# Opening an attention stage: the second pair of heads stacked by transfers, the first head's scores in four banks

## The reference

```python
B, H, S, D = (4, 8, 576, 64)
scores = scale * q @ k.T                      # per head, causal mask
a = softmax(scores)                           # rows reduced by their own maximum
local = a @ v
q_p = where(q > 0, q, exp(q) - 1) + 1
mem_out = (q_p @ M_prev) / (q_p @ z_prev + 1e-6)
g = sigmoid(beta)
x = (g * mem_out + (1 - g) * local)           # 2304 tokens x 512
x = (s * relu(x @ w_in)**2 + b) @ w_out       # 512 -> 2048 -> 512
h = x @ w_in2                                 # 512 -> 1024
x = layernorm(h * softmax(h)) * g_ln @ w_out2 # 1024 -> 512
```

## Time and profile before

| | us |
|---|---|
| median of three runs | 821.64 (821.0 to 822.66) |
| profiled execution | 821.17 |
| span of the profiled execution | 819.4 |
| PE busy | 810.7 (99%) |
| DVE busy | 510.4 (62%) |
| ACT busy | 339.6 (41%) |
| POOL busy | 339.1 (41%) |

### The profile page before, as it was taken

The page is one execution under the profiler, slowest core; times in us unless marked ns, Lnnn a source line. Parts: engine busy times, 40 slices in busy tenths (PEclk is TensorE's granted clock), DMA queues, the critical chain, the costliest instruction groups (busy, mean ns, idle before and its releaser), DMA issues.

```text
span 819.4 us, 14574 instructions
## 1 busy us (share of the span) xinstructions
PE 810.7 (99%) x5630; PEld 704.2 (86%) x5630; DVE 510.4 (62%) x1052; ACT 339.6 (41%) x608; POOL 339.1 (41%) x453
## 2 busy tenths in 40 slices
PE   8999999999999999999999999999999999999998
PEld 7788888888888888888888899999998888888886
DVE  7877777776588653333433353346688977777762
ACT  6766776675422232222322232233436434333431
POOL 6667676676899930000000000005268844443300
PEclk9999999999999999999999999999999999999999
DMA  8587777866134320000000000000111000000001
GB/s 152 128 178 154 173 167 155 178 142 144 53 103 116 95 73 1 1 1 0 1 1 0 1 1 1 1 1 1 52 51 52 26 27 26 26 14 27 26 14 51
DMA packets 86371, 49.45 MB, mean 60 GB/s; under 512 B 65056, under 2 KB 73248, under 8 KB 86304
## 3 DMA queue, kind: packets, MB, share of 16 engines
q1 hardware_dynamic: 83760, 47.94, 24.3%
q10 hardware_dynamic: 2544, 0.59, 0.4%
HBM read 27.28 MB, written 4.72 MB: 39 GB/s over the span
## 4 chain that ended last, share of the span: by engine, by line
PE 96%; DVE 1%; issue 0%; ACT 0%; POOL 0%; POOLq 0%
PE ps_h L1297 8%; PE ps_y L1313 8%; PE ps_h L1298 8%; PE ps_h L1299 8%; PE ps_y L1314 8%; PE ps_y L1312 8%; PE ps_v L678 5%; PE ps_s L591 4%; PE ps_r L1766 4%; PE ps_r L1764 4%; PE ps_r L1765 4%; PE ps_hid L1701 4%; PE ps_hid L1699 4%; PE ps_hid L1700 3%; PE ps_x L657 3%; PE ps_x L658 3%
## 5 line engine op out<-in xcount | busy, mean ns | idle before, releaser
L1414 DVE TENSOR_TENSOR xT<-xT 128x512 f32<-128x512 f32 (+1 forms) x80 | 61.2, 765 | 127.7 <-ACT xT L1372 127.7
L1598 POOL TENSOR_TENSOR win<-stage,win 128x512 fp32r<-128x512 f32 x2 | 2.6, 1296 | 282.4 <-ACT win L1833 282.4
L1314 PE MATMUL ps_y<-g_hi,wout 128*128 128x512 f32 (+1 forms) x320 | 117.5, 367 | 0.0
L1313 PE MATMUL ps_y<-g_lo,wout 128*128 128x512 f32 (+1 forms) x320 | 117.5, 367 | 0.0
L1312 PE MATMUL ps_y<-g_hi,wout 128*128 128x512 f32 (+1 forms) x320 | 117.4, 367 | 0.0
L1378 ACT ACTIVATE g_hi<-xT 128x512 fp32r<-128x512 f32 (+1 forms) x80 | 47.3, 591 | 135.0 <-DVE xT L1416 135.0
L1297 PE MATMUL ps_h<-x_hi,win 128*128 128x512 f32 (+1 forms) x280 | 103.0, 368 | 0.0
L1299 PE MATMUL ps_h<-x_hi,win 128*128 128x512 f32 (+1 forms) x280 | 102.8, 367 | 0.0
L1298 PE MATMUL ps_h<-x_lo,win 128*128 128x512 f32 (+1 forms) x280 | 102.8, 367 | 0.0
L1372 ACT ACTIVATE xT<-ps_h 128x512 f32<-128x512 f32 (+1 forms) x80 | 44.3, 554 | 139.0 <-PE ps_h L1299 137.2
L1419 DVE TENSOR_TENSOR g_lo<-xT,g_hi 128x512 fp32r<-128x512 f32 (+1 forms) x80 | 65.1, 813 | 52.6 <-ACT g_hi L1378 52.6
(11 more groups left out here) (220 smaller groups left out, 1814.6 us busy)
## 6 DMA issues: line engine op xcount, KB each, us to landing
stacked<-cut SPq DMA_DIRECT2D x56, 288.0 KB, 4.8
out<-res SPq DMA_DIRECT2D x18, 256.0 KB, 2.0
v_raw<-in_v SPq DMA_DIRECT2D x32, 128.0 KB, 2.7
stage<-in_moe_w_in SPq DMA_DIRECT2D x16, 256.0 KB, 2.8
stage<-in_moe_w_out SPq DMA_DIRECT2D x16, 256.0 KB, 2.7
k_raw<-in_k SPq DMA_DIRECT2D x28, 128.0 KB, 2.6
q_raw<-in_q SPq DMA_DIRECT2D x28, 128.0 KB, 3.6
stage<-in_moe_w_in SPq DMA_DIRECT2D x4, 512.0 KB, 3.5
```

The costliest lines, as they stand in the source:

```text
L1313: pe.matmul(out, wout[:, f, HI, w], g_lo[:, r, 0:n], start=False, stop=False)
L1314: ins = pe.matmul(out, wout[:, f, LO, w], g_hi[:, r, 0:n], start=False, stop=(f == FT - 1))
L1414: dve.tensor_tensor(r, r, r, ALU.mult).then_inc(square_done, 1)
```

## The change

Pair 1 is no longer placed directly (`DIRECT = 1`). Its keys and queries are loaded into the ordinary raw tiles, rounded by ScalarE and GpSimd, cut by VectorE and GpSimd, and brought to `stacked` by `stack(1)`, which SyncE issues behind the values of pair 0. The doubling on GpSimd and the swapped transposes of pair 1 are gone.

All rows of head 0 are computed in one go: tiles 4 and 1 in `ps_s` as before, tile 3 in the first bank of `ps_x`, tiles 0 and 2 in the second, without waits on maxima between them. Head 1's first rows follow as soon as their place in `ps_s` has been reduced. The transpose of head 0's maxima is taken out of `first_rows(1)` and has its own signal; head 1's low queries move from VectorE to GpSimd. GpSimd rounds and cuts pair 1's queries ahead of `spread_maxima(0)`, and a clearing of 1.53 us (the ones of `K1`) is moved behind it. ScalarE gets `round_keys(1)` and two `repeat_queries` for pair 1 in place of eight placing copies; VectorE's `work_out_gates` moves behind the first rows of head 1. Left out below: the same functions with their pair argument taken away, and sizes of counters.

```diff
--- before.py
+++ after.py
@@ -164,9 +164,8 @@
     Q1, K1 = sb("Q1", [P, SLOTS, 2, W], F32R), sb("K1", [P, LATE, 2, W], F32R)
     pT = [sb(f"pT{s}", [P, NP]) for s in range(3)]
     THREE = NT * 3 * D
-    first_k, first_q = ([words_.rearrange("p (t three d) -> p t three d", three=3, d=D) for words_ in places]
-                        for places in ((pT[0][:, 0:THREE], all_t_mem[:, 0:THREE]),
-                                       (pT[1][:, 0:THREE], all_t_mem[:, THREE:2 * THREE])))
+    first_k, first_q = (words_[:, 0:THREE].rearrange("p (t three d) -> p t three d", three=3, d=D)
+                        for words_ in (pT[0], pT[1]))
     rm, rl = sb("rm", [P, NT, 2]), sb("rl", [P, 2, NT])
...
@@ -180,6 +179,7 @@
         return ps_v[:, :, :].rearrange("p two n -> p (two n)") if p < 2 else ps_t
 
     S_AT = [512, 512 + REST, 512 + P, 0, 0]
+    X_AT = {3: (0, 0), 0: (1, 0), 2: (1, P)}
     NEG_AT = 512 + REST + 2 * P
 
...
@@ -218,12 +218,10 @@
     def is_head(h):
         return 0 <= h < HEADS
 
-    DIRECT = 2
-    BY_ACT = [(0, "k_own0"), (0, "k_moved0"), (0, "q_hi0"), (0, "q_cut0"), (0, "q_hi1"), (0, "q_own1"),
-              (1, "k_moved0"), (1, "k_moved1"), (1, "k_own0"), (1, "q_hi0"), (1, "q_cut0"), (1, "q_hi1"),
-              (1, "k_own1"), (1, "q_own1")]
-    BY_DVE = [(0, "k_own1"), (0, "k_moved1"), (0, "q_lo0"), (0, "q_lo1"), (1, "q_lo0")]
-    K_SWAPPED, Q_SWAPPED = (1, 3), (2, 4)
+    DIRECT = 1
+    BY_ACT = ["k_own0", "k_moved0", "q_hi0", "q_cut0", "q_hi1", "q_own1"]
+    BY_DVE = ["k_own1", "k_moved1", "q_lo0"]
+    K_SWAPPED, Q_SWAPPED = 1, 2
     Q_DMAS, STACK_DMAS = 3, 2
     MINE = [slice(0, D), slice(D, P)]
...
+    def score_rows(h, t):
+
+        if h == 0 and t in X_AT:
+            bank, at = X_AT[t]
+            return ps_x[:, bank, at:at + keys[t]]
+        return ps_s[:, S_AT[t]:S_AT[t] + keys[t]]
 
...
@@ -313,6 +315,7 @@
         load_queries(2)
         load_memory()
         load_values(0)
+        stack(1)
         load_keys(3)
         load_queries(3)
         load_values(1)
...
@@ -358,25 +361,22 @@
             for s in range(1, SLOTS):
                 pool.memset(words(Q1[MINE[0], s, 1, :]), 0.0).then_inc(cleared, 1)
             pool.memset(words(K1[:, 1:LATE, :, S:W]), 0.0).then_inc(cleared, 1)
+            pool.wait_ge(cleared, POOL_CLEARS - 1)
+
+        def fill_others():
...
+            pool.wait_ge(cleared, POOL_CLEARS - 1)
+
+        def fill_others():
             pool.memset(words(K1[MINE[0], 1:LATE, 1, 0:S]), 1.0).then_inc(cleared, 1)
             pool.wait_ge(cleared, POOL_CLEARS)
 
-        def double(raw, landed):
-
-            pool.wait_ge(landed, 16 * Q_DMAS)
-            pool.wait_ge(cleared_dve, PSUM_CLEARS)
-            pool.tensor_scalar(raw[:, :, 2, :], raw[:, :, 0, :], 1.0, 1.0, ALU.mult, ALU.mult).then_inc(doubled_pool, 1)
-
-        def repeat_first(p):
-            act_placed(pool, p, "q_hi0")
-            pool.tensor_scalar(Q1[MINE[0], p, 0, 0:S], words(stacked[MINE[0], slot(2 * p), 0, 0:S]), 1.0, 1.0,
+        def repeat_first():
+            act_placed(pool, "q_hi0")
+            pool.tensor_scalar(Q1[MINE[0], 0, 0, 0:S], words(stacked[MINE[0], slot(0), 0, 0:S]), 1.0, 1.0,
                                ALU.mult, ALU.mult).then_inc(repeated, 1)
 
         def low_queries():
 
-            act_placed(pool, 1, "q_own1")
-            pool.wait_ge(qT_copied, 2)
-            pool.tensor_tensor(stacked[MINE[1], slot(3), 0, 0:S], qT[1][MINE[1], :], Q1[MINE[1], 1, 1, 0:S],
+            act_placed(pool, "q_own1")
+            pool.wait_ge(qT_copied, 1)
+            pool.tensor_tensor(stacked[MINE[1], slot(1), 0, 0:S], qT[0][MINE[1], :], Q1[MINE[1], 0, 1, 0:S],
                                ALU.subtract).then_inc(low_by_pool, 1)
 
         def round_queries(p):
@@ -449,17 +449,16 @@
                 if even and is_pair(pr + 1):
                     features(pr + 1)
 
-        double(first_k[1], k_in[1])
-        double(first_q[1], q_in[1])
-        pool.wait_ge(doubled_pool, 2)
-        repeat_first(0)
+        repeat_first()
         pool.wait_ge(repeated, 1)
         clear_others()
-        repeat_first(1)
-        pool.wait_ge(repeated, DIRECT)
-        spread_maxima(0)
         low_queries()
         pool.wait_ge(low_by_pool, 1)
+        round_queries(1)
+        cut_queries(1)
+        pool.wait_ge(q_lo_done, 1)
+        spread_maxima(0)
+        fill_others()
 
         mask_weights(0, 0)
         pool.wait_ge(tri_done, 2)
@@ -523,37 +522,35 @@
...
+        def turn_maxima(h):
+            need(pe, maxed, 4 * (h + 1))
+            return pe.transpose(ps_s[:, NEG_AT:NEG_AT + P], least[h % 2][:, :], ident[:, :])
 
         def first_rows(h):
             if h == 0:
                 pe.wait_ge(cleared, FOR_ROWS)
-            if h < 2 * DIRECT:
-                p = h // 2
-                if h == 0:
-                    act_placed(pe, 0, "q_hi1")
-                    dve_placed(pe, 0, "q_lo0")
-                elif h == 1:
-                    act_placed(pe, 0, "q_hi1")
-                    dve_placed(pe, 0, "q_lo1")
-                elif h == 2:
-                    act_placed(pe, 1, "q_cut0")
-                    dve_placed(pe, 1, "q_lo0")
-                else:
-                    act_placed(pe, 1, "q_own1")
-                    pe.wait_ge(low_by_pool, 1)
+                act_placed(pe, "q_hi1")
+                dve_placed(pe, "q_lo0")
+            elif h == 1:
+                act_placed(pe, "q_own1")
+                pe.wait_ge(low_by_pool, 1)
+                pe.wait_ge(maxed, 2)
             elif h < HEADS:
                 p = h // 2
                 pe.wait_ge(stack_landed[p % SLOTS][h % 2], 16 * STACK_DMAS * stacks_sent(p))
-            need(pe, maxed, 4 * min(h, HEADS))
-            if is_head(h - 1):
-                ins = pe.transpose(ps_s[:, NEG_AT:NEG_AT + P], least[(h - 1) % 2][:, :], ident[:, :])
+            if is_head(h - 1) and h != 1:
+                ins = turn_maxima(h - 1)
             if h < HEADS:
                 rows_of_scores(h, 4)
                 ins = rows_of_scores(h, 1)
-            ins.then_inc(scored, 1)
+            if h != 1:
+                ins.then_inc(scored, 1)
 
         def second_rows(h):
-            pe.wait_ge(maxed, 4 * h + 1)
+            need(pe, maxed, 4 * h + 1 if h > 0 else 0)
             rows_of_scores(h, 3).then_inc(scored, 1)
 
         def third_rows(h):
-            pe.wait_ge(maxed, 4 * h + 2)
+            need(pe, maxed, 4 * h + 2 if h > 0 else 0)
             need(pe, neg_done, h)
             rows_of_scores(h, 0)
             rows_of_scores(h, 2).then_inc(scored, 1)
@@ -634,9 +628,7 @@
             a, p, par = slot(h), h // 2, h % 2
             kept = KEPT[par]
             if h == 0 and c == 0:
-                pe.wait_ge(k_lo_done, 1)
-                act_placed(pe, 1, "q_hi1")
-                dve_placed(pe, 1, "q_lo0")
+                pe.wait_ge(maxed, 4)
                 pe.wait_ge(cleared, FOR_FIRST)
                 pe.wait_ge(cleared_dve, DVE_CLEARS + 1)
             if h == 2 and c == 0:
...
@@ -730,25 +722,23 @@
 
         warm_up()
         turn_keys(0)
-        turn_swapped_keys(0)
+        turn_swapped_keys()
         turn_queries(0)
-        turn_swapped_queries(0)
-        act_placed(pe, 0, "k_moved0")
-        dve_placed(pe, 0, "k_moved1")
+        turn_swapped_queries()
+        act_placed(pe, "k_moved0")
+        dve_placed(pe, "k_moved1")
         keep_warm(ps_x[:, 0, 0:P])
         first_rows(0)
-        turn_swapped_keys(1)
-        pe.wait_ge(qT_copied, 1)
-        keep_warm(ps_t[:, 0:P])
         second_rows(0)
+        third_rows(0)
+        turn_queries(1)
         turn_keys(1)
-        turn_queries(1)
-        third_rows(0)
-        turn_swapped_queries(1)
-
         first_rows(1)
-        act_placed(pe, 1, "q_hi1")
-        keep_warm(ps_x[MINE[0], 0, 0:P], 4)
+        pe.wait_ge(qT_copied, 2)
+        keep_warm(ps_t[:, 0:P], 3)
+        turn_maxima(0).then_inc(scored, 1)
+        keep_warm(ps_t[:, 0:P], 4)
+
         cross(0, 0)
         second_rows(1)
         cross(0, 1)
...
-        for p, what in BY_ACT:
-            put(p, what)
-            if what == "q_own1":
-                copy_queries(p)
-                if p == 0:
-                    open_gates()
+        for what in BY_ACT:
+            put(what)
+        copy_queries(0)
+        open_gates()
+        copy_queries(1)
+        round_keys(1)
+        feature_relu(0)
         exp_weights(0, 0)
-        feature_relu(0)
+        repeat_queries(1, 0)
         exp_weights(0, 1)
         copy_queries(2)
         exp_weights(0, 2)
         feature_exp(0)
         exp_weights(0, 3)
+        repeat_queries(1, 1)
         round_keys(2)
 
         exp_weights(1, 0)
@@ -973,9 +963,8 @@
...
@@ -1128,24 +1113,24 @@
                     scale_local(pr - 1)
 
         dve.wait_ge(cleared_dve, DVE_CLEARS + 1)
-        double(first_k[0], k_in[0])
-        double(first_q[0], q_in[0])
+        double(first_k, k_in[0])
```

(75 more changed lines are left out.)

80 lines of the change are left out of this document (35 added, 45 removed).

## The result

The changed kernel takes 824.11 us (median of 11 executions, 822.58 to 827.92), the kernel before 821.43 us; the ratio is 1.0034 with a 95% interval of 1.0025 to 1.0042. It is 2.7 us slower. The profiled execution took 824.23 us, its span 822.3 against 819.4.

What follows compares the result with a forecast made beforehand. TensorE's queue plus the opening's holes was taken as the bound. The 1.7 us gained vanish in the wait for pair 1's stack, which adds 0.9: profiled 821.17 becomes 822.1, on the median 822.5 us; 8-in-10 range 821.2 to 824.9.

Steps and rivals of the forecast that it cites:

- the likeliest case: Whole kernel: pair 1's stack delays TensorE by 0.9 us, clock stays up, median 822.5 us; chance 0.50.
- the first rival: TensorE's clock falls in the 2.75 us hole, costing 1.4 us more: 823.9 us, range 823.0 to 825.0; chance 0.30.
- What bounds the kernel: TensorE's queue of work plus few holes in the opening; opening changes pay only if the unbroken queue starts at another moment.
- T: Turn of head 1's maxima with head 2's first rows on TensorE: 20.75 us before, forecast 21.65, bounds 21.3 and 22.4.
- The opening up to the first cross product: Head 0's rows, maxima and spreading: its cross product starts at 16.25 us, 1.7 us earlier.
- The new wait: TensorE waits for pair 1's first two transfers, issued by SyncE at 16.24 us; turn of head 1's maxima 0.9 us later.
- the landing: Pair 1's first two transfers, issue to landing: 5.1 us plus 0.2 for loads under way; upper bound 5.97 + 0.2.
- After T: Behind the turn of head 1's maxima, holes keep their distance; stack 2 issued at 28.25 us, in time; cost nothing.
- The two copies added to ScalarE: Query copies, about 0.65 us each, in ScalarE's idle time around the hole: cost nothing, without that cover up to 0.5 us.

Runs made afterwards that it cites:

- the run without a stack: Changed kernel without pair 1's stack, places of heads 2 and 3 cleared early by GpSimd and used as they are; 820.10 us, ratio 0.9982 to the kernel before.
- the early stack: Changed kernel with ScalarE rounding and VectorE subtracting pair 1's queries, its stack issued ahead of pair 0's values; 824.89 us, ratio 1.0043.
- the eight fillers: Changed kernel with eight filling matmuls in TensorE's wait for pair 1's stack; 823.03 us, ratio 1.0020.
- the half stack: Changed kernel with half of pair 1's stack copied by ScalarE on its own partitions, one transfer per head left; 821.41 us, ratio 1.0007.
- the turn of the maxima apart: Kernel before, with only the transpose of head 0's maxima given its own signal and head 1's first rows behind VectorE's copy; 821.28 us, ratio 0.9996.
- twelve: Changed kernel with twelve filling matmuls in TensorE's wait for pair 1's stack; 823.64 us, ratio 1.0026.
- three or two in the half stacks: Half of pair 1's transfers with three fillers, 821.34 us; or with two, queries ready earlier, stack ahead of values, head 3's copies later, 820.13 us.
- the early stack with five: Changed kernel with pair 1's queries readied by ScalarE and VectorE, stack ahead of values, and five filling matmuls; 822.35 us, ratio 1.0016.
- the stack ahead of the values: Changed kernel with one line moved: pair 1's stack issued ahead of the loads of pair 0's values; 825.46 us, ratio 1.0048.

## Why the prediction was right or wrong

The range held the time and the direction was right, but the likeliest case was not the one that came: it said 0.9 us, measured are 2.7. What came is the first rival, and its 823.9 us against the measured 824.11 is in part luck: the landing was longer than in its sum, the price of the clock lower, and 0.3 us came from elsewhere.

*What bounds the kernel.* Right. The later T appeared at the end one for one (2.56 us at head 3's turn, 2.87 at the last turn, 2.9 of span), and so did the earlier one in the run without a stack.

*The opening up to the first cross product.* Right in mechanism and nearly in size: 16.25 forecast, 16.36 measured; counted from head 0's rows, 5.82 and 6.11 us. The 0.3 us lie between the start of the spreading and the cross product, 1.06 us instead of 0.79: the 0.79 was read at head 1, while at head 0 itself the old kernel had 1.21 us, from the row below to 17.95.

```profile
16.74 0.74 POOL L404 TENSOR_SCALAR_AFFINE_SELECT Q<-negT 5x640 fp32r<-5x640 f32 x1 [0.97 <-DVE negT L1018]
```

That GpSimd's new operations of pair 1, and not the turned maxima, hold back the spreading is in its timeline (rounding, subtraction, then the spreading at once); the maxima had been copied since 14.81:

```profile
13.06 0.67 POOL L386 TENSOR_SCALAR cut<-qT 128x576 fp32r<-128x576 f32 x1
13.82 1.41 POOL L392 TENSOR_TENSOR cut<-qT,cut 128x576 fp32r<-128x576 f32 x1
15.30 0.74 POOL L404 TENSOR_SCALAR_AFFINE_SELECT Q<-negT 5x640 fp32r<-5x640 f32 x1
```

In the early stack, where GpSimd doesn't have these two operations, the cross product came 5.81 us behind head 0's rows instead of 6.11. The 1.7 us of gain were 1.5 when measured alone (1.41 by the distance of T from head 0's rows).

*The new wait.* Right in mechanism: SyncE's queue sets the issue (15.75; the stretch of loads ahead of it ended 0.5 us sooner than in the kernel before), TensorE waits on the second transfer. The term that was mis-sized is the landing: 5.1 + 0.2 us were taken and 5.97 + 0.2 was the upper bound, 6.6 came. The bound was made from the stacks of a single trace. What the traces have for this stack is 5.07 us where nothing stood just ahead, 5.0, 5.4 and 6.6 with the values ahead, 6.3 with the memory's transfers, whose last issue ended 0.8 us ahead. What makes the difference stays open: later stacks that were issued 0.1 us behind a load of keys took 5.06 us in the changed kernel (at 42.84) and 6.3 us with the eight fillers (at 41.13), and the one of 6.5 us in the changed kernel had 1.1 us free ahead of it. So the 0.2 us should have been a spread of 0 to 1.5. By the estimate from the Trainium skill ("DMA: Bandwidth & Descriptors", section "Anatomy of one DMA"), 3.4 us for both transfers, the miss would have been larger.

*After T.* The distances between T and what follows were kept within 0.1 us, as forecast, where the clock stayed up; the half stack, with its two more copies, lost the 0.4 us told above. The two copies added to ScalarE cost nothing. The prediction put that down to the hole as cover, without which they could cost up to 0.5 us; but the kernel without a stack has no hole at T, has both copies and keeps its lead, so they needed no cover. Stack 2 was issued at 29.19 us (28.25 forecast) and its second transfer landed 5.1 us later, in time for 36.31. Later in the attention 0.3 us were added, 0.2 of which is a wait of TensorE on the low parts of keys from VectorE; the sum had nothing for it. Between the second turn and the last the other traces have anything from -0.2 us (the turn of the maxima apart, no stack) to +0.45 us (eight fillers) against the kernel before, so it can't be put down to the change.

*The clock.* The step that failed is the choice between the forecast and the first rival. The hole became 3.3 us long because the landing was later, and the clock fell in the profiled execution and, by their mean clocks, in most of the others; the price was taken as 1.4 us and measured as 1.0 in the trace and 1.1 in the medians. The hole of 2.3 us at the end of the old kernel's span was a fair warning: a chance of 0.30 was small for a hole of 2.75 us. The Trainium skill ("TensorE: Matmul & The Clock Gate", section "HAM oscillation") tells of waits on transfers after which the next burst of matmuls starts at half rate. The trace agrees for the hole of 3.34 us (0.50 behind it); but the page tells it of longer waits than the forecast 2.75 us, so the prediction's sentence that by that rule the rival is what happens says more than the page does. The runs add that shorter holes are not safe either. In the early stack, with a hole of 2.0 us in the trace, it fell in all five executions (the traced one was the fastest, so the others' holes may have been longer); in the half stack, with 0.55 us in the trace, in two of eleven. With fillers in the hole it fell in none of 42 executions of four kernels (twelve, eight, and three or two in the half stacks), but in four of eleven of the early stack with five. Why there and not in the others is open.

## What to carry to other kernels

A producer that is moved from engines to a transfer queue must be timed from its place in that queue and with the whole spread of its landing, over several traces, and not from how long the same transfer takes elsewhere in one. Gains ahead of such a wait are worth nothing until the wait ends earlier than the old path did, and a hole on TensorE can cost, beside its length, a stretch at the lower clock, which fillers in it took away in most of these kernels, though not in all executions. Before moving one load ahead of another, find when each is wanted: here stack, values and memory were all wanted within about 6 us, no order of the three was faster than the kernel before, and what was faster had fewer bytes to move (a copy on an idle engine in place of half of the transfers) together with an earlier start.

## What the runs showed of the hardware

- The granted clock can fall after TensorE has resumed: in the changed kernel the hole ended at 22.36 us, the clock was 1.00 up to 22.4, 0.50 from 22.5 to 25.8 and 1.00 from 25.9. In the kernel with the early stack it stayed low for 6.8 us although TensorE was busy 6.48 us of them. With the stack ahead of the values it fell within the wait, 0.5 us ahead of its end.
- Two queued transfers of 288 KB between partitions took mostly 5.0 to 5.1 us from the first issue to the second landing, but up to 6.6 us in the opening and up to 6.5 us later; the first of the opening's took 3.3 to 4.1 us from its issue.
